# High and low parts of the last half key tiles share one product: nine products for a chunk instead of ten

## The chip, the core and the metric

The kernel runs on one core of a Trainium2 chip. Its time is the device time of one execution in microseconds (us), and the number that counts is the median of several runs. The engines are called PE (TensorE, matmuls), DVE (VectorE), ACT (ScalarE), POOL (GpSimd) and SP (SyncE, which issues DMAs here).

## The reference: what is computed

Attention with a threshold over 4 batches of 8 heads, 576 tokens and 64 columns a head, then two layers of a network over all 2304 tokens:

```python
scores = scale * q @ k.T                      # 576 x 576 for each head
thresh = max(scores) - tau                    # of each row
scores = where(scores >= thresh, scores, -1e9)
attn = softmax(scores)
x = attn @ v                                  # 576 x 64 for each head
x = relu(x @ w_in) ** 2 @ w_out               # 512 -> 2048 -> 512
h = x @ w2_in;  out = (h * tanh(softplus(h))) @ w2_out
```

## The kernel before

Numbers are float32. PE multiplies in a reduced form of it (`F32R`), so an operand is split: a high part, rounded to that form, and a low part, the rest. A product of two split operands is then three or four matmuls (high by high, high by low, and so on), all summed in PSUM.

**Slots.** The program is one list of slots, and every engine walks through it in order with its own share of each slot; semaphores tie them together. Two heads (a pair) have 9 query tiles of 128 rows, so there are 16 pairs and 144 tiles. Slot s computes the scores of tile s+1, the exponentials and the row maxima of tile s, the mask of tile s-1, and the transposes of tile s-3. From slot 40 on the first layer runs in the same slots: a slot has one `first_product` (12 matmuls, into the single PSUM tile `hidden`) and the `second_product` of the step two slots before (12 matmuls). The table `STEP_AT` leaves out one slot in nine, so in every nine slots there is one without a first product (slots 48, 57, 66, ..., 138; slot 39 has no product at all), called a **gap slot** here, and two slots later one without a second product (slots 50, 59, ..., 140, and slot 41 as the first of them), called a **half slot**.

**Order within a slot on PE:** transposes of tile s-3, first product, second product, scores, and in four slots of nine `weigh(c)`, the product of the transposed probabilities with the values for a chunk of 256 or 320 queries. There are 64 chunks, four to a pair. The first 16 (batch 0) go another way, with whole values in `weigh_whole`; the other 48 go through `weigh`. Both a gap slot and a half slot come right behind a slot that weighs a chunk of 256 queries.

**Transposed probabilities.** The 576 keys are covered by five tiles of 128 columns. The last but one holds keys 384 to 511 and the last keys 448 to 575, so that the lower 64 rows of the last tile repeat keys that the one before already has; the values for these rows are zero. PE transposes the five into one PSUM tile `pT`. ACT copies `pT` into the high part `pt_hi` (`high_probs`), then DVE subtracts it from `pT` into `pt_lo` (`low_probs`), 128x640 each. `transposes` of the next tile waits for that (`pT_low`), since it writes `pT` again. The values are split too, and `v_split` holds their high part in 64 columns and their low part in the next 64, so one matmul with `v_split` as the stationary operand gives both; the lower 64 rows of the result in `outs` belong to the high part and the upper 64 to the low part. ACT copies the upper ones to `o_low` (`move_low_rows`), DVE adds them (`sum_rows`) and SP stores the sum.

**Order on ACT in a slot:** the copy of `outs`, `high_probs`, `exponential`, in some slots the high parts of keys, queries and values, then `rectify` (`rg<-hidden` in the rows) and `high_square`, and sometimes `high_x`. `rectify` frees `hidden`: the next `first_product` waits for it (`relu_ready`). In a half slot ACT splits keys (`k_hi`) and values (`v_split`) ahead of `rectify`.

**Order on DVE:** row maxima (`s_neg`), `sum_rows`, mask (`probs<-s_neg,thresh,probs`), five small ones, `low_probs`, sometimes `low_x`.

In the rows, L562 is the helper of all ACT copies; L788 is `low_probs`, L796 `sum_rows`, L935 the transposes, L964 and L965 the two matmuls of `weigh`, L596 the exponential, L636 `rectify`, L642 `high_square`, L130 to L132 the three matmuls of each split product of the layers.

## Time and profile before

| | |
|---|---|
| median of 3 runs | 1150.06 us (1149.76 to 1151.54) |
| the profiled execution: its time, its span | 1150.88 us, 1149.1 us |
| mean granted TensorE clock | 0.994 of full speed |
| PE busy | 1105.6 us, 96% of the span |
| weight loads of PE | 1040.9 us, 91% |
| DVE, ACT, POOL busy | 759.2 us (66%), 645.4 us (56%), 586.2 us (51%) |
| PE's share of the chain that ended last | 86% |

A busy PE in this profile is not PE at its peak, since matmuls overlap in it: what a matmul costs is read from the distance between the starts of two that follow one another. The execution has three stages: batch 0 alone (to about 127 us), the other three batches beside the first layer (127 to 590 us), and the layers alone. The change bears on the second stage.

### The profile page before, as it was taken

The page shows a single profiled execution, that of the slowest core. Times are in us where ns is not written, and L with a number is a line of the kernel's source. Part 1 is how long each engine was busy: PE and PEld are TensorE (multiplying, and loading weights), DVE is VectorE, ACT ScalarE, POOL GpSimd, SP SyncE. Part 2 cuts the span into 40 slices and gives each one's busy share as a digit, 9 for nine tenths or more (in the row PEclk, how much of TensorE's full clock was granted, in tenths as well). Part 3 has the DMA queues.
Part 4 walks back from the last instruction along what each step waited for, and adds up shares of the span by engine and source line. Part 5 has one row for each costly group of instructions (what it writes and reads, how often), then busy time and mean ns, then how long its engine had stood idle before and what let it go on. Part 6 is the DMA issues. An engine that isn't in the chain of part 4 may idle for free.

```text
span 1149.1 us, 21018 instructions
## 1 busy us (share of the span) xinstructions
PE 1105.6 (96%) x7472; PEld 1040.9 (91%) x7472; DVE 759.2 (66%) x1977; ACT 645.4 (56%) x1230; POOL 586.2 (51%) x657
## 2 busy tenths in 40 slices
PE   5998899999999999999999999899999999999998
PEld 4776799999999999999999999889999999999997
DVE  5776677777677667676631014588787777878775
ACT  5786566665656566656543236555555555555554
POOL 5887788666766677676644445322222222222222
PEclk9999999999999999999999999999999999999999
DMA  5454322112222212121010204500101001010000
GB/s 147 130 153 113 92 74 72 53 49 70 55 71 58 60 47 81 44 69 53 20 50 11 92 2 146 156 19 1 56 1 56 1 1 56 1 55 1 28 1 28
DMA packets 73545, 65.33 MB, mean 57 GB/s; under 512 B 26080, under 2 KB 58848, under 8 KB 73440
## 3 DMA queue, kind: packets, MB, share of 16 engines
q1 hardware_dynamic: 68528, 58.98, 17.9%
q10 hardware_dynamic: 4912, 5.01, 1.3%
q8 instruction: 59, 0.97, 0.4%
q14 instruction: 46, 0.38, 0.1%
HBM read 49.81 MB, written 14.16 MB: 56 GB/s over the span
## 4 chain that ended last, share of the span: by engine, by line
PE 86%; DVE 4%; ACT 4%; issue 2%; DMA 2%; POOL 1%; SPq 0%; POOLq 0%; ACTq 0%; DVEq 0%
PE acc L130 8%; PE acc L131 8%; PE acc L132 8%; PE hidden L130 7%; PE hidden L132 7%; PE hidden L131 7%; PE pT L935 6%; PE scores L130 3%; PE scores L132 3%; PE scores L131 3%; PE pT L130 3%; PE pT L132 3%; PE pT L131 3%; PE outs L964 3%; PE outs L965 3%; PE scores L924 3%
## 5 line engine op out<-in xcount | busy, mean ns | idle before, releaser
L531 POOL TENSOR_TENSOR g_lo<-g,g_hi 128x384 fp32r<-128x384 f32 x96 | 97.9, 1020 | 314.0 <-ACT g_hi L562 314.0
L505 POOL TENSOR_SCALAR probs<-probs,inv_sum,flat 128x576 f32<-128x576 f32 x144 | 120.6, 839 | 130.8 <-DVE inv_sum L781 130.5
L130 PE MATMUL hidden<-x_hi,w_hi 128*128 128x256 f32 x576 | 170.6, 296 | 2.3 <-DVE x_lo L806 1.6
L130 PE MATMUL acc<-g_hi,w_hi 128*128 128x256 f32 x576 | 163.9, 285 | 0.2 <-POOL g_lo L526 0.2
L131 PE MATMUL acc<-g_lo,w_hi 128*128 128x256 f32 x576 | 162.9, 283 | 0.0
L132 PE MATMUL acc<-g_hi,w_lo 128*128 128x256 f32 x576 | 162.8, 283 | 0.0
L132 PE MATMUL hidden<-x_hi,w_lo 128*128 128x256 f32 x576 | 162.7, 282 | 0.0
L131 PE MATMUL hidden<-x_lo,w_hi 128*128 128x256 f32 x576 | 162.5, 282 | 0.0
L745 DVE TENSOR_SCALAR_CACHE_REDUCE s_neg<-scores 128x576 f32<-128x576 f32 x126 | 95.0, 754 | 71.5 <-PE scores L925 71.3
L521 POOL TENSOR_TENSOR rg<-rg 128x256 f32<-128x256 f32 x144 | 98.4, 683 | 75.4 <-ACT rg L636 74.5
L562 ACT ACTIVATE pt_hi<-pT 128x640 fp32r<-128x640 f32 x108 | 76.3, 707 | 71.0 <-PE pT L935 67.4
L596 ACT ACTIVATE probs<-s_neg,neg_top 128x576 f32<-128x576 f32 x144 | 110.5, 767 | 9.3 <-DVE s_neg L745 9.0
L562 ACT ACTIVATE g_hi<-g 128x384 fp32r<-128x384 f32 x96 | 50.5, 526 | 113.6 <-DVE g L847 113.6
L526 POOL TENSOR_TENSOR g_lo<-rg,g_hi 128x256 fp32r<-128x256 f32 x144 | 107.9, 749 | 11.3
L130 PEld LDWEIGHTS hidden<-x_hi,w_hi 128*128 128x128 f32 x576 | 109.8, 191 | 3.1 <-DVE x_lo L806 2.0
L935 PE MATMUL pT<-ident,probs 128*128 128x128 f32 x720 | 103.6, 275 | 9.3 <-DVE pt_lo L788 6.1
L130 PEld LDWEIGHTS acc<-g_hi,w_hi 128*128 128x128 f32 x576 | 110.4, 192 | 0.4 <-POOL g_lo L526 0.4
L131 PEld LDWEIGHTS acc<-g_lo,w_hi 128*128 128x128 f32 x576 | 110.5, 192 | 0.0
L132 PEld LDWEIGHTS acc<-g_hi,w_lo 128*128 128x128 f32 x576 | 110.4, 192 | 0.0
L131 PEld LDWEIGHTS hidden<-x_lo,w_hi 128*128 128x128 f32 x576 | 110.0, 191 | 0.0
L132 PEld LDWEIGHTS hidden<-x_hi,w_lo 128*128 128x128 f32 x576 | 109.7, 190 | 0.0
L935 PEld LDWEIGHTS pT<-ident,probs 128*128 128x128 f32 x720 | 84.3, 141 | 19.9 <-issue 9.8
(116 smaller groups left out, 3106.5 us busy)
## 6 DMA issues: line engine op xcount, KB each, us to landing
k_raw<-kT SPq DMA_DIRECT2D x64, 144.0 KB, 2.9
q_raw<-qT SPq DMA_DIRECT2D x62, 144.0 KB, 3.0
y<-w_in SPq DMA_DIRECT2D x26, 256.0 KB, 2.8
y<-w_out SPq DMA_DIRECT2D x26, 256.0 KB, 3.1
x_raw<-x SPq DMA_DIRECT2D x36, 128.0 KB, 2.1
x<-y ACTq DMA_DIRECT2D x9, 512.0 KB, 2.9
x_raw<-x SPq DMA_DIRECT2D x6, 768.0 KB, 5.1
out<-y SPq DMA_DIRECT2D x18, 256.0 KB, 2.4
```

The lines of the kernel that those rows point to most:

```text
L130: pe.matmul(out, a_hi, b_hi, start=first, stop=False, **flags)
L131: pe.matmul(out, a_hi, b_lo, start=False, stop=False, **flags)
L132: return pe.matmul(out, a_lo, b_hi, start=False, stop=last, **flags)
L505: pool.tensor_scalar(probs[:, t, :], probs[:, t, :], inv_sum[:, t:t + 1], flat[:, t:t + 1], ALU.mult, ALU.add).then_inc(probs_ready, 1)
L521: pool.tensor_tensor(g[:, i % 2, :], r[:, i % 2, :], r[:, i % 2, :], ALU.mult).then_inc(g_ready, 1)
L526: pool.tensor_tensor(g_lo[:, i % GRING1, :], g[:, i % 2, :], g_hi[:, i % GRING1, :].bitcast(F32), ALU.subtract).then_inc(g_split, 1)
L531: pool.tensor_tensor(g2_lo[:, k % GRING, :], g2[:, k % 2, :], g2_hi[:, k % GRING, :].bitcast(F32), ALU.subtract).then_inc(g2_split, 1)
L562: return act.activation(o, i, ACT.Copy)
L596: act.activation(probs[:, t, :], s_neg[:, n % 2, :], ACT.Exp, bias=neg_top[:, t:t + 1], scale=-1.0).then_inc(exp_ready, 1)
L745: dve.tensor_scalar(s_neg[:, n % 2, :].rearrange("p (c k) -> p c k", c=2), scores_of(n)[:, :, 0:HALF], -SCALE, None, ALU.mult, ALU.min, ac ...
L924: pe.matmul(out, q, k_hi[:, u, keys], start=(u, at) == parts[0], stop=False)
L935: mm = pe.transpose(pT[:, k * P:(k + 1) * P], probs[:, n % PRING, tile_at(k):tile_at(k) + P], ident[:, :])
```

## The change

From chunk 16 on the four matmuls of the last two key tiles become three. The fourth key tile is now the last one (keys 448 to 575, `BOTH`), the fifth keys 384 to 511 (`LAST`). The high part of `BOTH` is not multiplied any more, and neither is the low part of `LAST` as a tile; in their place one product takes a mixed tile, which has the low part of keys 384 to 447 in its lower 64 rows and the high part of keys 512 to 575 in its upper 64 rows, with a sixth block of values in the same order. For that:

- DVE writes `pt_lo` with two instructions, 128x512 and 64x128, instead of one of 128x640;
- ACT copies the upper 64 rows of the high part of `BOTH` into `pt_lo` (64x128), with a semaphore of its own, `pT_moved`, on which `weigh` waits; it first waits for its own copy to `pt_hi`;
- values have six blocks instead of five: ACT's and POOL's part of `v_split` are 128x384 instead of 128x320, and SP issues four DMAs a head for them instead of two;
- `o_low` and `o_sum` become `o_moved` and `o_sum` of 128 rows, in which the chunks take turns between lower and upper rows.

```diff
-                for k in range(QT):
-                    values = v_split[:, c // 2 % 2, k, :]
-                    pe.matmul(outs[:, 0:w], values, pt_hi[:, k, at:at + w], start=(k == 0), stop=False)
-                    mm = pe.matmul(outs[:, 0:w], values, pt_lo[:, k, at:at + w], start=False,
-                                   stop=(k == QT - 1))
+                for k, (_, place) in enumerate(KEY_TILES):
+                    values = v_split[:, c // 2 % 2, place, :]
+                    if k != BOTH:
+                        pe.matmul(outs[:, 0:w], values, pt_hi[:, k, at:at + w], start=(k == 0), stop=False)
+                    if k != LAST:
+                        pe.matmul(outs[:, 0:w], values, pt_lo[:, k, at:at + w], start=False, stop=False)
+
+                values = v_split[:, c // 2 % 2, QT, :]
+                mm = pe.matmul(outs[:, 0:w], values, pt_lo[:, LAST, at:at + w], start=False, stop=True)
                 mm.then_inc(out_ready, 1)
...
                 copy(pt_hi[:, :, at:at + P], pT_tile).then_inc(pT_high, 1)
+                if n == WHOLE_TILES:
+                    act.wait_ge(out_ready, WHOLE_CHUNKS)
+                act.wait_ge(pT_high, n + 1)
+                copy(pt_lo[HD:P, LAST, at:at + P], pt_hi[HD:P, BOTH, at:at + P].bitcast(F32)).then_inc(pT_moved, 1)
...
-                dve.tensor_tensor(pt_lo[:, :, at:at + P], pT_tile, pt_hi[:, :, at:at + P].bitcast(F32),
-                                  ALU.subtract).then_inc(pT_low, 1)
+                dve.tensor_tensor(pt_lo[:, 0:LAST, at:at + P], pT_tile[:, 0:LAST, :],
+                                  pt_hi[:, 0:LAST, at:at + P].bitcast(F32), ALU.subtract)
+                dve.tensor_tensor(pt_lo[0:HD, LAST, at:at + P], pT_tile[0:HD, LAST, :],
+                                  pt_hi[0:HD, LAST, at:at + P].bitcast(F32), ALU.subtract).then_inc(pT_low, 1)
...
-                copy(v_split[:, h % 2, :, 0:HD], v_raw[:, h % 2, 0:QT, :]).then_inc(v_high, 1)
+                copy(v_split[:, h % 2, :, 0:HD], v_raw[:, h % 2, :, :]).then_inc(v_high, 1)
...
-                sp.dma_start(v_raw[HD:P, h % 2, QT - 1, :], v[h * SEQ + 512:(h + 1) * SEQ, :]
-                             ).then_inc(v_loaded[h % 2], 16)
+                if h < HEADS:
+                    sp.dma_start(v_raw[HD:P, h % 2, QT - 1, :], v[h * SEQ + 512:(h + 1) * SEQ, :]
+                                 ).then_inc(v_loaded[h % 2], 16)
+                else:
+                    sp.dma_start(v_raw[:, h % 2, QT - 1, :], v[h * SEQ + 448:(h + 1) * SEQ, :]
+                                 ).then_inc(v_loaded[h % 2], 16)
+                    sp.dma_start(v_raw[0:HD, h % 2, QT, :], v[h * SEQ + 384:h * SEQ + 448, :]
+                                 ).then_inc(v_loaded[h % 2], 16)
+                    sp.dma_start(v_raw[HD:P, h % 2, QT, :], v[h * SEQ + 512:(h + 1) * SEQ, :]
+                                 ).then_inc(v_loaded[h % 2], 16)
```

What ACT has to do in a half slot (slot 59), before; the line numbers of the changed program are other ones, L562 becomes L586, L596 becomes L620, L636 and L642 become L664 and L670:

```order
L562 ACTIVATE o_low<-outs 64x256
L562 ACTIVATE pt_hi<-pT 128x5x128
L596 ACTIVATE probs<-s_neg,neg_top 128x576
L562 ACTIVATE k_hi<-k_raw 128x576
L562 ACTIVATE v_split<-v_raw 128x5x64
L636 ACTIVATE rg<-hidden 128x256
L642 ACTIVATE g_hi<-rg 128x256
```

And the same slot on ACT in the changed kernel:

```order
L586 ACTIVATE o_moved<-outs 64x256
L586 ACTIVATE pt_hi<-pT 128x5x128
L586 ACTIVATE pt_lo<-pt_hi 64x128
L620 ACTIVATE probs<-s_neg,neg_top 128x576
L586 ACTIVATE k_hi<-k_raw 128x576
L586 ACTIVATE v_split<-v_raw 128x6x64
L664 ACTIVATE rg<-hidden 128x256
L670 ACTIVATE g_hi<-rg 128x256
```

One instruction more stands between `pt_hi` and the exponential, ahead of `rg<-hidden`, and `v_split` is longer.

PE in a slot that weighs a chunk of 256, from `weigh` to the transposes behind it, before:

```order
L964 MATMUL outs<-pt_hi,v_split 128x256
L965 MATMUL outs<-pt_lo,v_split 128x256
L964 MATMUL outs<-pt_hi,v_split 128x256
L965 MATMUL outs<-pt_lo,v_split 128x256
L964 MATMUL outs<-pt_hi,v_split 128x256
L965 MATMUL outs<-pt_lo,v_split 128x256
L964 MATMUL outs<-pt_hi,v_split 128x256
L965 MATMUL outs<-pt_lo,v_split 128x256
L964 MATMUL outs<-pt_hi,v_split 128x256
L965 MATMUL outs<-pt_lo,v_split 128x256
L935 MATMUL pT<-ident,probs 128x128 x5
```

And in the changed kernel, where L1001 is the product of the mixed tile:

```order
L996 MATMUL outs<-pt_hi,v_split 128x256
L998 MATMUL outs<-pt_lo,v_split 128x256
L996 MATMUL outs<-pt_hi,v_split 128x256
L998 MATMUL outs<-pt_lo,v_split 128x256
L996 MATMUL outs<-pt_hi,v_split 128x256
L998 MATMUL outs<-pt_lo,v_split 128x256 x2
L996 MATMUL outs<-pt_hi,v_split 128x256
L1001 MATMUL outs<-pt_lo,v_split 128x256
L965 MATMUL pT<-ident,probs 128x128 x5
```

Nine instead of ten, and nothing else on PE changes its place.

## Rows read from the trace of the kernel before

**Rows 1.** Engines in the second stage: length, then busy us and instructions of each
```profile
127.00:590.00 463.00, 456.40 (x3736) 451.62 (x3735) 322.86 (x1012) 280.55 (x548) 325.90 (x370) 1.00 0.21 57
```

**Rows 2.** What PE waited for in that stage: us in total, times, longest
```profile
PE pT L935 <- DVE pt_lo L788: 5.4, 13, 0.4
```

**Rows 3.** Timeline of PE, from the weighing in slot 58 through half slot 59
```profile
207.28 0.28 PE L964 MATMUL outs<-pt_hi,v_split 128*128 128x256 f32 x1
...
208.47 0.71 PE L935 MATMUL pT<-ident,probs 128*128 128x128 f32 x5
...
211.56 0.74 PE L935 MATMUL pT<-ident,probs 128*128 128x128 f32 x5 [0.43 <-DVE pt_lo L788]
212.05 0.36 PE L130 MATMUL hidden<-x_hi,w_hi 128*128 128x256 f32 x1
```

**Rows 4.** Timeline of PE: a chunk of 320 and the transposes behind it
```profile
307.00 0.31 PE L964 MATMUL outs<-pt_hi,v_split 128*128 128x320 f32 x1
...
308.46 0.71 PE L935 MATMUL pT<-ident,probs 128*128 128x128 f32 x5
```

**Rows 5.** Timeline of ACT in half slot 59
```profile
209.21 0.70 ACT L562 ACTIVATE pt_hi<-pT 128x640 fp32r<-128x640 f32 x1 [0.17 <-PE pT L935]
209.82 0.76 ACT L596 ACTIVATE probs<-s_neg,neg_top 128x576 f32<-128x576 f32 x1
...
211.06 0.46 ACT L562 ACTIVATE v_split<-v_raw 128x320 fp32r<-128x320 f32 x1
211.42 0.37 ACT L636 ACTIVATE rg<-hidden 128x256 f32<-128x256 f32 x1
211.82 0.42 ACT L642 ACTIVATE g_hi<-rg 128x256 fp32r<-128x256 f32 x1
```

**Rows 6.** Timeline of DVE in half slot 59
```profile
210.60 0.81 DVE L788 TENSOR_TENSOR pt_lo<-pT,pt_hi 128x640 fp32r<-128x640 f32 x1
211.33 0.75 DVE L745 TENSOR_SCALAR_CACHE_REDUCE s_neg<-scores 128x576 f32<-128x576 f32 x1
```

**Rows 7.** Groups by line and shape, second stage: busy us, mean ns
```profile
L499 POOL TENSOR_TENSOR v_split<-v_raw,v_split 128x320 fp32r<-128x320 f32 x23 | 29.8, 1296 | 0.9
...
L796 DVE TENSOR_TENSOR o_sum<-outs,o_low 64x320 f32<-64x320 f32 x24 | 11.6, 483 | 29.6 <-ACT o_low L562 29.6
L562 ACT ACTIVATE v_split<-v_raw 128x320 fp32r<-128x320 f32 x23 | 10.6, 459 | 0.0
...
L562 ACT ACTIVATE x_hi<-x_raw 128x256 fp32r<-128x256 f32 x24 | 9.7, 402 | 0.0
L796 DVE TENSOR_TENSOR o_sum<-outs,o_low 64x256 f32<-64x256 f32 x23 | 9.6, 417 | 20.9 <-ACT o_low L562 20.9
```

**Rows 8.** Timeline of gap slot 57: transposes, the low part, the next transposes
```profile
200.23 0.71 PE L935 MATMUL pT<-ident,probs 128*128 128x128 f32 x5
...
202.37 0.81 DVE L788 TENSOR_TENSOR pt_lo<-pT,pt_hi 128x640 fp32r<-128x640 f32 x1
...
203.32 0.74 PE L935 MATMUL pT<-ident,probs 128*128 128x128 f32 x5
```

**Rows 9.** Timelines of ACT and PE, end of half slot 41
```profile
132.77 0.37 ACT L636 ACTIVATE rg<-hidden 128x256 f32<-128x256 f32 x1
...
133.28 0.36 PE L130 MATMUL hidden<-x_hi,w_hi 128*128 128x256 f32 x1 [0.58 <-ACT rg L636]
```

**Rows 10.** Timelines of DVE and PE around the end of slot 53
```profile
184.30 0.81 DVE L788 TENSOR_TENSOR pt_lo<-pT,pt_hi 128x640 fp32r<-128x640 f32 x1
...
185.78 0.71 PE L935 MATMUL pT<-ident,probs 128*128 128x128 f32 x5
```

**Rows 11.** Timelines of ACT and PE around the end of slot 55
```profile
194.12 0.37 ACT L636 ACTIVATE rg<-hidden 128x256 f32<-128x256 f32 x1
...
195.57 0.36 PE L130 MATMUL hidden<-x_hi,w_hi 128*128 128x256 f32 x1
```

**Rows 12.** Instructions on v_raw: duration ns min/median/max, first and last start
```profile
L364 SPq DMA_DIRECT2D v_raw<-v x32: 511/517/813, 3.1 to 527.8; - x32
```

More of the change, by code:

```diff
@@ L66 @@
 SLOTS = BEGIN2 + NB * FT + LEAD + 1
-def tile_at(k):
-    return min(k * P, SEQ - P)
+KEY_TILES = [(0, 0), (P, 1), (2 * P, 2), (SEQ - P, 4), (3 * P, 3)]
+BOTH, LAST = 3, 4
 def chunk_ended(n):
@@ L175, in attention_and_layers @@
         k_lo = early("k_lo", [P, 2, SEQ], F32R)
-        v_split = early("v_split", [P, 2, QT, 2 * HD], F32R)
+        v_split = early("v_split", [P, 2, QT + 1, 2 * HD], F32R)
         s_neg = early("s_neg", [P, 2, SEQ])
         probs = early("probs", [P, PRING, SEQ])
-        o_low = early("o_low", [HD, 320])
-        o_sum = early("o_sum", [HD, 2, 320])
+        o_moved = early("o_moved", [P, 320])
+        o_sum = early("o_sum", [P, 320])
         ident = early("ident", [P, P])
@@ L235, in scores_of, with rows_of, other_rows @@
             return both_acc if n < WHOLE_TILES and n % 2 else scores
+        def rows_of(c):
+            return slice(c % 2 * HD, (c % 2 + 1) * HD)
+        def other_rows(c):
+            return slice((c + 1) % 2 * HD, ((c + 1) % 2 + 1) * HD)
         def outs_of(c):
@@ L279, in attention_and_layers @@
         pT_low = sem("pT_low")
+        pT_moved = sem("pT_moved")
         out_ready = sem("out_ready")
-        low_moved = sem("low_moved")
+        rows_moved = sem("rows_moved")
         out_summed = sem("out_summed")
@@ L318, in w_tile, with values_loaded @@
             return w[:, f * 2 * DM:(f + 1) * 2 * DM]
+        def values_loaded(h):
+            return 32 * (h // 2 + 1) + 32 * max(0, (h - HEADS) // 2 + 1)
         def query_columns(h):
@@ L371, in store @@
                 at = h // HEADS * SEQ
-                o = o_sum[:, c % 2, :]
+                o = o_sum[rows_of(c), :]
                 if c % 4 == 0:
@@ L498, in split_values @@
                 pool.wait_ge(v_high, h + 1 - HEADS)
-                pool.tensor_tensor(v_split[:, h % 2, :, HD:2 * HD], v_raw[:, h % 2, 0:QT, :],
+                pool.tensor_tensor(v_split[:, h % 2, :, HD:2 * HD], v_raw[:, h % 2, :, :],
                                    v_split[:, h % 2, :, 0:HD].bitcast(F32), ALU.subtract).then_inc(v_ready, 1)
@@ L622, in move_low_rows @@
                 act.wait_ge(out_summed, c)
-                copy(o_low[:, 0:w], outs[HD:P, 0:w]).then_inc(low_moved, 1)
+                copy(o_moved[rows_of(c), 0:w], outs[other_rows(c), 0:w]).then_inc(rows_moved, 1)
             def copy_rows(c):
@@ L629, in copy_rows @@
                 act.wait_ge(out_ready, c + 1)
-                copy(o_sum[:, c % 2, 0:w], outs_of(c)[0:HD, 0:w]).then_inc(out_summed, 1)
+                copy(o_sum[rows_of(c), 0:w], outs_of(c)[0:HD, 0:w]).then_inc(out_summed, 1)
             def rectify(i):
@@ L700, in _ @@
                 if c is not None and c >= WHOLE_CHUNKS:
[L701 removed]
+                    move_rows(c)
                 if 0 <= s - LAG < WHOLE_TILES:
@@ L794, in sum_rows @@
                     dve.wait_ge(stored[c % 2], stored_up_to(c - 1, c % 2))
-                dve.wait_ge(low_moved, c + 1 - WHOLE_CHUNKS)
-                dve.tensor_tensor(o_sum[:, c % 2, 0:w], outs[0:HD, 0:w], o_low[:, 0:w], ALU.add
+                dve.wait_ge(rows_moved, c + 1 - WHOLE_CHUNKS)
+                dve.tensor_tensor(o_sum[rows_of(c), 0:w], outs[rows_of(c), 0:w], o_moved[rows_of(c), 0:w], ALU.add
                                   ).then_inc(out_summed, 1)
@@ L933, in transposes @@
                     pe.wait_ge(pT_low, n - WHOLE_TILES)
-                for k in range(QT):
-                    mm = pe.transpose(pT[:, k * P:(k + 1) * P],
-                                      probs[:, n % PRING, tile_at(k):tile_at(k) + P], ident[:, :])
+                for k, (key, _) in enumerate(KEY_TILES):
+                    mm = pe.transpose(pT[:, k * P:(k + 1) * P], probs[:, n % PRING, key:key + P], ident[:, :])
                 mm.then_inc(pT_ready, 1)
@@ L951, in weigh_whole @@
                 for k in keys:
-                    mm = pe.matmul(outs_of(c)[:, 0:w], values[:, k * HD:k * HD + P], pt_whole[c % 2][:, k, 0:w],
+                    at = KEY_TILES[k][1] * HD
+                    mm = pe.matmul(outs_of(c)[:, 0:w], values[:, at:at + P], pt_whole[c % 2][:, k, 0:w],
                                    start=(k == 0), stop=(k == QT - 1))
@@ L960, in weigh @@
                 pe.wait_ge(pT_low, PER * (c // 4) + last + 1 - WHOLE_TILES)
+                pe.wait_ge(pT_moved, PER * (c // 4) + last + 1 - WHOLE_TILES)
                 pe.wait_ge(v_ready, c // 2 + 1 - HEADS)
-                for k in range(QT):
-                    values = v_split[:, c // 2 % 2, k, :]
-                    pe.matmul(outs[:, 0:w], values, pt_hi[:, k, at:at + w], start=(k == 0), stop=False)
-                    mm = pe.matmul(outs[:, 0:w], values, pt_lo[:, k, at:at + w], start=False,
-                                   stop=(k == QT - 1))
+                for k, (_, place) in enumerate(KEY_TILES):
[6 more added lines that the diff above has]
+                mm = pe.matmul(outs[:, 0:w], values, pt_lo[:, LAST, at:at + w], start=False, stop=True)
                 mm.then_inc(out_ready, 1)
```

7 lines of the change are left out of this document (3 added, 4 removed).

## The prediction, made before the changed kernel ran

> **What bounds the kernel now.** I read the busy time by stage first. In the second stage PE is busy for 456.4 of 463.0 us [rows 1], with the granted clock at 1.00, while DVE (322.9), ACT (280.6) and POOL (325.9) have a third of it free. So PE's own work sets the pace. The waits come next: PE waits 5.4 us in 13 places for the low part `pt_lo` of the transposed probabilities [rows 2], 0.43 us in each of the 12 half slots as in [rows 3], 5.2 us together, and 0.2 once more. Last the timelines, which show what stands beside PE in the places where it doesn't set the pace. There are two kinds. In a half slot PE has no second product, and its transposes start only when `pt_lo` has ended: 210.60 + 0.81 = 211.41 [rows 6], transposes at 211.56 [rows 3], 0.15 us later, of which I take 0.14 as the way of a semaphore. In a gap slot it is the same without a recorded wait: `pt_lo` ends at 202.37 + 0.81 = 203.18, transposes at 203.32, again 0.14 us later [rows 8]. In both, the chain runs from the end of the weighing before (ACT copies `outs`, DVE adds, masks, and then subtracts), so its start moves with the weighing, and a shorter weighing is kept. A longer `pt_lo` is paid in full there. In all other slots PE is alone on the path.
>
> **What is saved.** One of ten products of `weigh`, 48 times. With 256 columns ten take 208.47 - 207.28 = 1.19 us [rows 3], 0.119 us each; with 320 columns 308.46 - 307.00 = 1.46 us [rows 4], 0.146 each. 24 chunks of each: 24 x 0.119 + 24 x 0.146 = 2.86 + 3.50 = 6.36 us. The nine have the same shapes, and each has its own weight load as before.
>
> **What DVE pays.** 640 columns in one instruction become 512 and 128 in two. The fixed part of a DVE subtraction or addition with a PSUM operand follows from `o_sum`: 417 ns at 256 columns, 483 at 320 [rows 7], so 1.03 ns a column and 153 ns fixed. The 64x128 one then takes 0.285 us and the 128x512 one 0.81 - 0.13 = 0.68. Two that follow each other overlap: `pt_lo` starts at 210.60, takes 0.81, and the next starts at 211.33 [rows 6], 0.08 us before its end. The pair takes 0.68 - 0.08 + 0.285 = 0.88 us instead of 0.81; with the exact halves (133 ns less for 128 columns) it is 0.06 to 0.07. I take 0.06. Bounds: 0 (a perfect overlap of the fixed part) and 0.153 (none). In the gap slots it is paid in full, 12 times with slot 39: 0.72 us. In the other slots it is hidden. The closest I found away from the two kinds is the end of slot 53, where `pt_lo` ends at 185.11 and the transposes start at 185.78 [rows 10], 0.53 us more than the semaphore needs.
>
 By that rule the gap slots would lose 12 x 0.125 = 1.5 us instead of 0.7, and the overlap in the trace speaks for the smaller value.
>
> **What ACT pays.** Every tile gets a copy of 64x128 from SBUF to SBUF. Its length from the two nearest rows: 402 ns at 256 columns (`x_hi`), 459 at 320 (`v_split`) [rows 7], so 0.89 ns a column and 402 - 114 = 288 ns; I take 0.29. It also waits for the copy to `pt_hi` ahead of it, and that ends the overlap: `pt_hi` starts at 209.21 and takes 0.70, the exponential starts at 209.82, 0.09 to 0.10 us before its end [rows 5]. With the wait the next starts 0.03 us after the end, as `g_hi` behind `rg` shows (211.42 + 0.37 = 211.79, start 211.82) [rows 5]. So the exponential and all behind it in the slot come 0.10 + 0.03 + 0.29 - 0.10 = 0.32 to 0.33 us later. In a half slot `v_split` is longer by 64 columns too, 0.055 us. Together 0.385 us.
>
> Who waits for that? In the half slot ACT works without a gap from `pt_hi` at 209.21 to the end of `rg` at 211.79 [rows 5], and the next first product needs `rg` to free `hidden`. It starts at 212.05 [rows 3]. That is 0.26 us after `rg`; from slot 41, where PE did wait for `rg`, such a start needs 0.14 (132.77 + 0.37 = 133.14, start 133.28) [rows 9]. So only 0.12 us of the 0.385 are free, and the first product starts 0.265 us later than now. This takes the place of the 0.06 of DVE there: the transposes come 0.06 later, but the first product behind them waits for `rg` anyway. In slot 41, which is late already, all of 0.385 is paid. 11 x 0.265 + 0.39 = 3.3 us. (The last, slot 140, has no keys to split, but a copy and low part of x before the next row maxima; I price it like the others.)
>
> In other slots the copy is hidden. The tightest after these is the end of slot 55: `rg` ends at 194.49, the first product starts at 195.57 [rows 11], 0.94 us more than 0.14. The exponential itself is needed by the mask one slot later.
>
> **What else moves.** POOL's part of `v_split` goes from 1.30 us [rows 7] to an estimated 1.56 for a fifth more columns; what it holds up is a square whose low part is due two slots later, and POOL is idle for a third of the stage. SP issues two DMAs more for each of 24 heads at 0.52 us [rows 12], so about 1 us later for what is behind them, in a queue that works one to three slots (3 us and more each) ahead. `o_moved` in place of `o_low` has the same shapes. The new wait of `weigh` on `pT_moved` is for an instruction near the start of the slot at whose end `weigh` stands, and earlier than the `pt_lo` for which it waits already. I cost these at nothing. Without their cover, a late POOL or SP would show as a wait of PE for `g_lo` or of ACT for a DMA.
>
> **The sum.** -6.36 + 0.72 + 3.3 = -2.3 us. The profiled execution took 1150.88 us, span 1149.1; it would take 1148.5, span 1146.8. The median shown is 0.8 us below the profiled time, so the median to come is 1150.06 - 2.3 = **1147.7 us**.
>
> **Rivals.**
> 1. *The saving is nearly whole.* If ACT's new copy were free in the half slots (shorter or overlapping, so that the delay stays under 0.12 us), only DVE's part is lost, 24 x 0.06 = 1.4 us: -4.9 us, 1145.1. For it: ACT is busy for 61% of the stage only. Against it: it has no gap in just these slots. With the copy at the least its rows allow, 402 - 256 x 0.89 = 174 ns (no time for its columns), the delay is 0.21 + 0.055, the loss there 0.145 x 11 + 0.27 = 1.9, and the sum -3.8: 1146.3.
> 2. *DVE's second instruction costs its whole fixed part,* 0.125 to 0.153 us. In the half slots the wait for `rg` covers it, in the gap slots it costs 12 x 0.09 = 1.1 us more at most: -1.2 us, 1148.8. The rule quoted above gives this case, at 12 x 0.065 = 0.8 us more, 1148.5.
> 3. *Slower: ACT's copy is as long as that of the whole tile.* If reading what was just written makes the 64x128 copy as long as `pt_hi`, 0.70 us, the delay in a half slot is 0.10 + 0.03 + 0.70 - 0.10 + 0.055 = 0.785, PE waits 0.665 longer in 11 and 0.785 in one: 8.1 + 0.7 - 6.36 = +2.4 us, 1152.5. It breaks even where 11 x (d - 0.12) + d = 5.64, at a delay d of 0.58 us, so at a copy of 0.49 us. For it: nothing in the trace is exactly this copy. Against it: all ACT copies follow one line by columns.
> 4. *PE saves nothing,* because nine products with the same output are not faster than ten. Nothing speaks for it, since their starts are evenly spaced and next in line is always a matmul.
>
> **How the numbers follow.** About 0.2% (2.3 us) is what a measurement of this kernel can tell from no change. My forecast lies just on that edge. Forecast (-1.6 to -3.1) 0.62; rival 1 0.14 (whole or in part); rival 2 0.12; rival 3 and everything else that makes ACT or a queue late 0.10; rival 4 0.02. The forecast's own range is 1147.0 to 1148.5. The range for 8 in 10 goes to rival 1 below and past rival 2 above: 1145.2 to 1149.6. Faster by over 0.2% is half of the forecast, rival 1 and nothing else, with a little more because parts of what I charge may overlap: 0.48. Within 0.2%: 0.45. Slower by over 0.2%: 0.07, from rival 3.
>
> **What would show it.** In the changed profile: `weigh` takes 9 x 0.119 and 9 x 0.146 us from its first start to the next transposes; `pt_lo` lasts 0.68 and 0.285 us, the second start some 0.6 after the first; ACT's new copy lasts 0.29 and the exponential starts about 0.93 us after `pt_hi` instead of 0.61. PE has a wait for `rg` in each of the 12 half slots, 0.2 us beyond its transposes and more in slot 41, where today there is one in all. From the transposes of a half slot to the next first product it is 3.84 us instead of 3.58 (212.05 - 208.47); from transposes to transposes in a gap slot 3.15 instead of 3.09. What makes me wrong: a new copy of another length, a chain that DVE finds late for another reason, above all its mask, which shares a slot with POOL's work, or a wait in a slot where I see none.

## The result, and the profile after

| | before | changed kernel |
|---|---|---|
| median | 1149.92 us (1149.23 to 1151.54, 6 runs) | 1156.02 us (1154.86 to 1157.84, 6 runs) |
| the profiled execution: its time, its span | 1150.88, 1149.1 | 1157.50, 1155.7 |

The ratio is 1.0048, with an interval of 1.0034 to 1.0062: the change makes the kernel 0.5% slower, where 0.2% faster was forecast. The one rival with that sign, a copy on ACT as long as that of the whole tile, isn't the reason either: the copy is as short as predicted.

The busy time by stage, as in [rows 1]; the middle line is the second stage.

```profile
0.00:127.00 127.00, 101.68 (x534) 81.74 (x534) 82.10 (x323) 86.58 (x138) 92.56 (x94) 0.97 0.48 135
127.00:590.00 463.00, 448.92 (x3637) 439.99 (x3637) 339.62 (x1122) 317.09 (x647) 325.27 (x366) 1.00 0.22 60
590.00:1155.70 565.70, 554.87 (x3256) 513.76 (x3254) 354.36 (x641) 282.91 (x555) 168.69 (x197) 1.00 0.12 39
```

In 463 us PE was busy for 456.4 us before and is for 448.9 now, with the clock at 1.00 in both. So PE waits more, and DVE (339.6 instead of 322.9) and ACT (317.1 instead of 280.6) work more. What PE waits for, as in [rows 2]: us in total, times, longest.

```profile
PE pT L965 <- POOL probs L529: 8.4, 23, 0.5
PE outs L996 <- issue: 3.0, 6, 0.5
PE hidden L134 <- ACT rg L664: 1.1, 1, 1.1
PE hidden L134 <- DVE x_lo L836: 0.8, 1, 0.8
PE pT L965 <- DVE pt_lo L818: 0.8, 1, 0.8
```

The 13 waits of the transposes have become 24. The first line names POOL, but its probabilities belong to the next tile's transposes as much as `pt_lo` does, both end close together, and the transposes start 0.15 us behind the end of `pt_lo`, as before. The wait for `rg` that the prediction announced for every half slot shows in one slot alone: in the others the transposes ahead of it are recorded as busy until the first product starts, so the delay shows only in the distance between starts. The second line is new in kind: `weigh` itself waits, in six places.

The lengths that the prediction used, by groups from 127 to 596 us, the end of the stage's last slots (busy us, mean ns | idle before):

```profile
L798 DVE SCALAR_TENSOR_TENSOR probs<-s_neg,thresh,probs 128x576 f32<-128x576 f32 x105 | 108.6, 1034 | 0.7
...
L816 DVE TENSOR_TENSOR pt_lo<-pT,pt_hi 128x512 fp32r<-128x512 f32 x107 | 72.5, 677 | 4.2 <-ACT pt_hi L586 3.5
L586 ACT ACTIVATE pt_lo<-pt_hi 64x128 fp32r<-64x128 f32 x107 | 32.9, 308 | 3.4
L523 POOL TENSOR_TENSOR v_split<-v_raw,v_split 128x384 fp32r<-128x384 f32 x23 | 29.9, 1300 | 0.9
L818 DVE TENSOR_TENSOR pt_lo<-pT,pt_hi 64x128 fp32r<-64x128 f32 x107 | 29.1, 272 | 0.0
```

ACT's copy takes 0.308 us (0.29 predicted), DVE's pair 0.677 and 0.272 (0.68 and 0.285). The surprise is the mask, which the change doesn't touch: 1.034 us on average, where it was 0.924.

**Where the time went, by slot.** I measured every slot from its transposes to the next, in both traces. From slot 39 to slot 146, the last with transposes, the sum is 6.2 us longer; slot 39 itself came 1.6 us later in this execution, and the rest of the span differs by 1.2 the other way. In us, by kinds of slots (slots after 48, with two typical lengths):

| slots | before, after | sum of the difference |
|---|---|---|
| half slot | 3.09, 3.14 | +0.5 |
| the slot behind it | 3.97, 4.25 | +3.1 |
| the next one, weighs 320 (11 slots) | 5.40, 5.25; but 6.03 in slots 52, 70, 88, 106, 124 | +2.2 |
| the other three kinds that weigh | 5.15, 5.04; 5.40, 5.25; 5.12, 5.00 | -3.9 |
| gap slot (10) | 3.09, 3.41 | +3.0 |
| the two kinds left | 3.94, 3.94 | +0.1 |
| slots 39 to 48 | | +1.2 |

The products are saved as predicted (0.12 and 0.15 us a chunk), and the half slots cost about what was predicted. Two rows are not as predicted: the gap slots, 0.32 us longer and not 0.06, and five slots in which 0.15 is not gained and 0.63 is lost.

**A gap slot.** Slot 66 in the kernel before, timeline of DVE and PE:

```profile
239.32 0.71 PE L935 MATMUL pT<-ident,probs 128*128 128x128 f32 x5
240.00 0.42 DVE L796 TENSOR_TENSOR o_sum<-outs,o_low 64x256 f32<-64x256 f32 x1 [0.90 <-ACT o_low L562]
240.34 0.80 DVE L770 SCALAR_TENSOR_TENSOR probs<-s_neg,thresh,probs 128x576 f32<-128x576 f32 x1
241.37 0.17 DVE L781 RECIPROCAL inv_sum<-safe_sum 128x1 f32<-128x1 f32 x1
241.45 0.81 DVE L788 TENSOR_TENSOR pt_lo<-pT,pt_hi 128x640 fp32r<-128x640 f32 x1
```

The same slot in the changed kernel:

```profile
242.81 0.71 PE L965 MATMUL pT<-ident,probs 128*128 128x128 f32 x5
243.49 0.43 DVE L826 TENSOR_TENSOR o_sum<-outs,o_moved 64x256 f32<-64x256 f32 x1 [0.78 <-ACT o_moved L586]
243.95 0.82 DVE L798 SCALAR_TENSOR_TENSOR probs<-s_neg,thresh,probs 128x576 f32<-128x576 f32 x1
245.00 0.17 DVE L809 RECIPROCAL inv_sum<-safe_sum 128x1 f32<-128x1 f32 x1
245.20 0.69 DVE L816 TENSOR_TENSOR pt_lo<-pT,pt_hi 128x512 fp32r<-128x512 f32 x1
245.81 0.27 DVE L818 TENSOR_TENSOR pt_lo<-pT,pt_hi 64x128 fp32r<-64x128 f32 x1
246.22 0.74 PE L965 MATMUL pT<-ident,probs 128*128 128x128 f32 x5 [0.22 <-POOL probs L529]
```

The mask starts 0.46 us behind the start of the addition instead of 0.34, and `pt_lo` 0.20 behind the reciprocal instead of 0.08. Both are 0.12 us, with no wait of DVE in the rows, and only where the addition works in the upper rows (odd chunks, as in every gap slot); behind even chunks the mask follows at 0.34 as before. With 0.06 for the pair and some hundredths in the masks and starts that is the 0.32. Put against the ends of the instructions ahead: before, the mask starts 0.08 us before the addition has ended (240.42) and `pt_lo` 0.09 before the reciprocal has (241.54); now both start 0.03 us behind such an end (243.92, 245.17).

**One of the five.** Slot 70 before, DVE and POOL:

```profile
254.12 0.74 POOL L526 TENSOR_TENSOR g_lo<-rg,g_hi 128x256 fp32r<-128x256 f32 x1
254.43 0.70 DVE L806 TENSOR_TENSOR x_lo<-x_raw,x_hi 128x256 fp32r<-128x256 f32 x1 [0.59 <-ACT x_hi L562]
254.63 0.71 PE L935 MATMUL pT<-ident,probs 128*128 128x128 f32 x5
...
255.73 0.81 DVE L770 SCALAR_TENSOR_TENSOR probs<-s_neg,thresh,probs 128x576 f32<-128x576 f32 x1
...
255.92 1.92 POOL L494 TENSOR_TENSOR q_split<-q_raw,q_split 64x576 fp32r<-64x576 f32 x1
...
258.56 0.31 PE L964 MATMUL outs<-pt_hi,v_split 128*128 128x320 f32 x1
```

And after:

```profile
258.64 0.71 PE L965 MATMUL pT<-ident,probs 128*128 128x128 f32 x5
...
258.92 0.42 DVE L836 TENSOR_TENSOR x_lo<-x_raw,x_hi 128x256 fp32r<-128x256 f32 x1 [1.21 <-ACT x_hi L586]
...
259.94 2.07 DVE L798 SCALAR_TENSOR_TENSOR probs<-s_neg,thresh,probs 128x576 f32<-128x576 f32 x1
259.96 1.43 POOL L518 TENSOR_TENSOR q_split<-q_raw,q_split 64x576 fp32r<-64x576 f32 x1
...
262.91 0.27 DVE L818 TENSOR_TENSOR pt_lo<-pT,pt_hi 64x128 fp32r<-64x128 f32 x1
...
263.28 0.39 PE L996 MATMUL outs<-pt_hi,v_split 128*128 128x320 f32 x1 [0.55 <-issue]
```

The mask starts 1.30 us behind the transposes instead of 1.10, because ACT, later by its copy, delivers `x_hi` later, and so DVE `x_lo` and the row maxima. `x_lo` starts 0.48 us later (0.28 behind the transposes, where it was 0.20 ahead of them), but only 0.20 of it reaches the mask: before, `x_lo` took 0.70 us beside POOL's `g_lo`, now it takes 0.42. Before, the mask was 0.19 us ahead of POOL's `q_split` and took 0.81 us, while POOL took 1.92. Now they start together, POOL takes 1.43 and the mask 2.07. It ends 0.62 us behind POOL's end (259.96 + 1.43 = 261.39; 259.94 + 2.07 = 262.01), as if it had 0.62 us of work to do from there. `pt_lo` then ends at 263.18, and `weigh` of this slot, which needs it, starts at 263.28.

### The profile page after: what moved, and what is told of

The parts are those of the page before. It is cut to its first block, busy times and chain, and to the rows that moved or that the text cites. A ratio compares the mean times of both kernels' runs of the same rounds, so it can differ in the third digit from the quotient of the medians.

```text
span 1155.7 us, 21235 instructions
## 1 busy us (share of the span) xinstructions
PE 1105.5 (96%) x7424; PEld 1035.5 (90%) x7424; DVE 776.1 (67%) x2085; ACT 686.6 (59%) x1338; POOL 586.5 (51%) x657
## 4 chain that ended last, share of the span: by engine, by line
PE 81%; DVE 5%; ACT 5%; POOL 4%; issue 3%; DMA 2%; SPq 0%; POOLq 0%; ACTq 0%; DVEq 0%
PE acc L134 7%; PE acc L135 7%; PE acc L136 7%; PE hidden L134 7%; PE hidden L136 7%; PE hidden L135 7%; PE pT L965 5%; PE pT L136 3%; PE pT L134 3%; PE pT L135 3%; PE scores L136 3%; PE scores L134 3%; PE scores L135 3%; PE outs L996 2%; PE outs L998 2%
## 5 line engine op out<-in xcount | busy, mean ns | idle before, releaser
L586 ACT ACTIVATE g_hi<-g 128x384 fp32r<-128x384 f32 x96 | 50.5, 526 | 113.6 <-DVE g L877 113.6
L620 ACT ACTIVATE probs<-s_neg,neg_top 128x576 f32<-128x576 f32 x144 | 111.6, 775 | 10.1 <-DVE s_neg L773 7.1
L798 DVE SCALAR_TENSOR_TENSOR probs<-s_neg,thresh,probs 128x576 f32<-128x576 f32 x108 | 111.2, 1030 | 0.7
L586 ACT ACTIVATE pt_hi<-pT 128x640 fp32r<-128x640 f32 x108 | 76.0, 703 | 52.9 <-PE pT L965 49.7
```

Source lines behind the costliest of these rows:

```text
L586: return act.activation(o, i, ACT.Copy)
L620: act.activation(probs[:, t, :], s_neg[:, n % 2, :], ACT.Exp, bias=neg_top[:, t:t + 1], scale=-1.0).then_inc(exp_ready, 1)
L798: dve.scalar_tensor_tensor(out=probs[:, t, :], in0=s_neg[:, n % 2, :], scalar=thresh[:, t:t + 1], in1=probs[:, t, :], op0=ALU.is_le, op1=A ...
```

## The experiments

All ratios are to the kernel before, run beside it on the same chip, and can differ a little from the quotient of the two medians. Sums over the second stage are made like those above (6.2 us in the changed kernel), from one profiled execution each; whole times scatter by 1 to 5 us between executions. Where an expectation speaks of a type, it means the number of the slot modulo nine: the gap slots are of type 3, the half slots of type 5, the slot behind them of type 6, the five long slots of type 7.

**1. Nine products alone**, on the kernel before. The low part of the last key tile is left out of the values' product, so the kernel does less than the reference asks.

```diff
-                    pe.matmul(outs[:, 0:w], values, pt_hi[:, k, at:at + w], start=(k == 0), stop=False)
-                    mm = pe.matmul(outs[:, 0:w], values, pt_lo[:, k, at:at + w], start=False,
+                    mm = pe.matmul(outs[:, 0:w], values, pt_hi[:, k, at:at + w], start=(k == 0),
                                    stop=(k == QT - 1))
+                    if k < QT - 1:
+                        pe.matmul(outs[:, 0:w], values, pt_lo[:, k, at:at + w], start=False, stop=False)
```

> The kernel before, with nine products a chunk from chunk 16 on and nothing else changed: the product with the low part of the last key tile is left out (so the output lacks that part). If a product costs what the starts of its neighbours show (0.119 us at 256 columns, 0.146 at 320), 48 of them save 6.4 us, 1143.5 us. If nine are not faster than ten, or a stall takes the place, 1149.9.

Measured: 1144.19 us against 1151.49, ratio 0.9938 [0.9925, 0.9952], stage sum -6.15. Slot 48 is 0.22 us longer in it (its mask takes 1.15 us instead of 0.92, beside POOL's work) and the others are 6.37 shorter, so the saving of 6.36 is right, and all of the loss is on the other side.

**2. The sum always in the lower rows**, in the changed kernel; all sums then share one buffer, so each addition waits for the store of the chunk before.

```diff
-            return slice(c % 2 * HD, (c % 2 + 1) * HD)
+            odd = c % 2 if c < WHOLE_CHUNKS else 0
+            return slice(odd * HD, (odd + 1) * HD)
...
-                if c >= 2:
-                    dve.wait_ge(stored[c % 2], stored_up_to(c - 1, c % 2))
+                for parity in range(2):
+                    dve.wait_ge(stored[parity], stored_up_to(c, parity))
```

> The changed kernel, but from chunk 16 on o_moved and o_sum always in the lower 64 rows (one buffer each, the sum waits for the store of the chunk before). Theory A, that a DVE addition on the upper 64 rows makes the instructions behind it later (mask 0.12 us, low part 0.11 us), which is paid in the 12 gap slots: 2.8 us less than the changed kernel, 1153.2 us, and gap slots 3.15 us long instead of 3.41. Theory B, that the gap slots are longer by the second DVE instruction or POOL: no change, 1156.0.

Measured: 1155.56 us, ratio 1.0034 [1.0021, 1.0046], stage sum +4.2 instead of +6.2. Gap slots take 3.17 instead of 3.41; nothing else moves much. So the rows of the addition cost 2 us, and the rest of the loss isn't theirs.

**3. ACT's copy late**, behind `rg`, `g_hi` and `x_hi` of its slot.

```diff
                 copy(pt_hi[:, :, at:at + P], pT_tile).then_inc(pT_high, 1)
+
+            def move_high(n):
+                at = COLUMN[n % PER]
...
                 if s in SPLIT_AT:
                     high_x(*SPLIT_AT[s])
+                if WHOLE_TILES <= s - LAG < TILES:
+                    move_high(s - LAG)
```

> The changed kernel with ACT's new 64x128 copy moved to the end of its share of the slot, behind rg, g_hi and x_hi. Theory A, that its place ahead of the exponential costs 0.33 us in each half slot (3.6 with slot 41) and, by making x_hi late, 0.78 us in each of five slots of type 7 of nine (3.9): 7.6 us less than the changed kernel, 1148.4 us. Theory B, that the place of the copy costs only the half slots and the five slots are long for another reason (POOL's longer value split, DMAs): 1152.4.

Measured: 1156.53 us, ratio 1.0044 [1.0031, 1.0056], stage sum +5.85. The half slots keep their 3.14 us, and the slots behind them are at 3.97 again as before the change, 3 us back. But the other kind of slot that weighs 320 queries (slots 54, 63, ..., 144) loses 0.28 us (5.53 instead of 5.25, eleven times): `weigh` needs the copy, which now ends 3.88 us behind the transposes in slot 63, and starts at 4.13 instead of 3.94, and slots 52 and 70 still take 6.15. My expectation took the copy's cover in the weighing slots for granted, and it isn't there: a step moved out of one slot kind landed on the path in another.

**4. `high_x` ahead of the queries' high part** on ACT, in the slots before the five, in the changed kernel.

```diff
+                if s in SPLIT_AT and s % PER == 6:
+                    high_x(*SPLIT_AT[s])
                 if s in QUERIES_AT:
                     high_queries(QUERIES_AT[s])
...
-                if s in SPLIT_AT:
+                if s in SPLIT_AT and s % PER != 6:
                     high_x(*SPLIT_AT[s])
```

> The changed kernel with high_x taken ahead of q_split on ACT in the slots of type 6 of nine alone. Theory A, that in five slots of type 7 the mask starts just as POOL's q_split does and lasts 2.07 us instead of 0.81 because x_hi, x_lo and the row maxima came 0.4 us later: the five long slots (6.03 us) go back to 5.25, 3.9 us less than the changed kernel, 1152.1. Theory B, that the long mask has to do with POOL or the DMAs of the values: no change, 1156.0.

Measured: 1152.53 us, ratio 1.0009 [1.0000, 1.0018], stage sum +2.4. The five slots take 5.25, all others what they took in the changed kernel. The masks start 0.17 to 0.23 us ahead of `q_split` again and take 0.81 us.

**5. The alternate rows alone**, on the kernel before (`o_low` and `o_sum` of 128 rows, odd chunks in the upper 64).

```diff
-                copy(o_low[:, 0:w], outs[HD:P, 0:w]).then_inc(low_moved, 1)
+                copy(o_low[rows_of(c), 0:w], outs[other_rows(c), 0:w]).then_inc(low_moved, 1)
...
-                dve.tensor_tensor(o_sum[:, c % 2, 0:w], outs[0:HD, 0:w], o_low[:, 0:w], ALU.add
+                dve.tensor_tensor(o_sum[rows_of(c), 0:w], outs[rows_of(c), 0:w], o_low[rows_of(c), 0:w], ALU.add
```

> The kernel before with one part of the change alone: o_low and o_sum hold 128 rows and the chunks take turns between lower and upper rows. Theory A (an addition on the upper rows delays what follows on DVE by 0.12 and 0.11 us, which 12 gap slots pay in full): +2.8 us against before, gap slots 3.32 us instead of 3.09. Theory B (only together with the second DVE instruction): no change.

Measured: 1155.85 us against 1151.44, ratio 1.0037 [1.0025, 1.0049], stage sum +3.8, of it 2.5 in ten gap slots (3.35), 0.8 in slot 48 and 0.5 in slots 40 and 45.

**6. ACT's copy alone**, on the kernel before, into a block of values that nothing reads.

```diff
                 copy(pt_hi[:, :, at:at + P], pT_tile).then_inc(pT_high, 1)
+                if n == WHOLE_TILES:
+                    act.wait_ge(out_ready, WHOLE_CHUNKS)
+                act.wait_ge(pT_high, n + 1)
+                copy(v_raw[HD:P, :, QT, :], pt_hi[HD:P, QT - 1, at:at + P].bitcast(F32).rearrange("p (a d) -> p a d", a=2))
```

> The kernel before with ACT's 64x128 copy of every tile alone, written to a block of v_raw that nobody reads any more. By the prediction's own sum the half slots pay 0.33 - 0.12 = 0.21 us each, 2.6 us in all. Theory A adds to that the late x_hi, which lets five masks coincide with POOL's q_split, up to 0.8 us each: 2.6 to 6.6 us. Theory B (the five slots have another cause): 2.6 us and no long slot of type 7.

Measured: 1156.35 us, ratio 1.0049 [1.0037, 1.0061], stage sum +5.4: +2.8 behind the half slots (4.25), +2.1 in the same five slots, 5.84 instead of 5.40, and +0.5 in slots 39 to 48. The copy alone brings both of its losses, 5 us and not 3.3. The second one comes about in another way than in the changed kernel. Slot 70, whose transposes start at 257.43, POOL and DVE:

```profile
257.48 0.82 POOL L505 TENSOR_SCALAR probs<-probs,inv_sum,flat 128x576 f32<-128x576 f32 x1
257.68 0.90 DVE L810 TENSOR_TENSOR x_lo<-x_raw,x_hi 128x256 fp32r<-128x256 f32 x1 [1.20 <-ACT x_hi L562]
...
259.18 1.31 DVE L774 SCALAR_TENSOR_TENSOR probs<-s_neg,thresh,probs 128x576 f32<-128x576 f32 x1
```

Here it is `x_lo` that comes together with POOL's work, and it takes 0.90 us instead of 0.42. The mask then starts 1.75 us behind the transposes, when POOL has been at `q_split` for 0.79 us, and takes 1.31.

**7. The low part in two instructions alone** (128x512 and 128x128), on the kernel before.

```diff
-                dve.tensor_tensor(pt_lo[:, :, at:at + P], pT_tile, pt_hi[:, :, at:at + P].bitcast(F32),
-                                  ALU.subtract).then_inc(pT_low, 1)
+                dve.tensor_tensor(pt_lo[:, 0:QT - 1, at:at + P], pT_tile[:, 0:QT - 1, :],
+                                  pt_hi[:, 0:QT - 1, at:at + P].bitcast(F32), ALU.subtract)
+                dve.tensor_tensor(pt_lo[:, QT - 1, at:at + P], pT_tile[:, QT - 1, :],
+                                  pt_hi[:, QT - 1, at:at + P].bitcast(F32), ALU.subtract).then_inc(pT_low, 1)
```

> The kernel before with low_probs in two instructions, 128x512 and 128x128, and nothing else. Both theories: 0.055 us in each of the 12 gap and 12 half slots, where transposes wait for it, +1.3 us. If the second instruction costs a whole fixed part (0.125 us or more), +3 us.

Measured: 1153.33 us, ratio 1.0017 [1.0008, 1.0025], stage sum +1.4: 0.06 us in each gap slot (3.15) and each half slot (3.15), as priced, but for slots 57 and 120, which take 3.28.

**8. and 9. Which rows?** Two halves of experiment 5 on the kernel before: only the output of odd sums in the upper rows, and only their inputs.

```diff
-                dve.tensor_tensor(o_sum[:, c % 2, 0:w], outs[0:HD, 0:w], o_low[:, 0:w], ALU.add
+                dve.tensor_tensor(o_sum[rows_of(c), 0:w], outs[0:HD, 0:w], o_low[0:HD, 0:w], ALU.add
...
-                dve.tensor_tensor(o_sum[:, c % 2, 0:w], outs[0:HD, 0:w], o_low[:, 0:w], ALU.add
+                dve.tensor_tensor(o_sum[sum_at(c), 0:w], outs[rows_of(c), 0:w], o_low[rows_of(c), 0:w], ALU.add
```

(`sum_at` gives the lower rows from the second batch on; in that half the addition also waits for the store of the chunk before.)

> The kernel before with the sum of odd chunks written to the upper 64 rows, and both inputs of the addition in the lower ones. If the delay behind the addition comes from where it writes, 12 gap slots are 3.35 us long as with all operands in the upper rows (3 to 4 us more than before); if it comes from where it reads, 3.09 us and no change.

> The kernel before with both inputs of the addition in the upper 64 rows for odd chunks, and the output always in the lower ones (one buffer, so the sum waits for the store of the chunk before). If the delay comes from where it reads, gap slots are 3.35 us long and the kernel is 3 to 4 us slower than before; if from where it writes, 3.09 to 3.12.

Measured: the output alone 1153.94 us against 1151.73, ratio 1.0015 [1.0007, 1.0024], stage sum +2.2, gap slots 3.22; the inputs alone 1154.50, ratio 1.0028 [1.0017, 1.0039], stage sum +4.4, gap slots 3.38. The expectations took it for one or the other; it is both. Slot 66 with only the output in the upper rows:

```profile
242.39 0.42 DVE L802 TENSOR_TENSOR o_sum<-outs,o_low 64x256 f32<-64x256 f32 x1 [0.90 <-ACT o_low L568]
242.84 0.82 DVE L776 SCALAR_TENSOR_TENSOR probs<-s_neg,thresh,probs 128x576 f32<-128x576 f32 x1
243.89 0.16 DVE L787 RECIPROCAL inv_sum<-safe_sum 128x1 f32<-128x1 f32 x1
243.97 0.80 DVE L794 TENSOR_TENSOR pt_lo<-pT,pt_hi 128x640 fp32r<-128x640 f32 x1
```

And with only the inputs there:

```profile
241.55 0.43 DVE L805 TENSOR_TENSOR o_sum<-outs,o_low 64x256 f32<-64x256 f32 x1 [0.92 <-ACT o_low L571]
242.01 0.82 DVE L779 SCALAR_TENSOR_TENSOR probs<-s_neg,thresh,probs 128x576 f32<-128x576 f32 x1
243.05 0.17 DVE L790 RECIPROCAL inv_sum<-safe_sum 128x1 f32<-128x1 f32 x1
243.25 0.82 DVE L797 TENSOR_TENSOR pt_lo<-pT,pt_hi 128x640 fp32r<-128x640 f32 x1
```

Both delay the mask (0.45 instead of 0.34 behind the addition). Only the inputs delay `pt_lo` too (0.20 instead of 0.08 behind the reciprocal). Between the two stand the mask and five small instructions, all in SBUF alone, and `pt_lo` is the next to read PSUM after the addition read its upper rows.

**10. POOL's low part of the queries later**, the changed kernel with one move on POOL: in the slots before the five, behind the square and its low part.

```diff
-                if s in QUERIES_AT:
+                if s in QUERIES_AT and s % PER != 6:
                     split_queries(QUERIES_AT[s], s)
...
                     low_square(i)
+                if s in QUERIES_AT and s % PER == 6:
+                    if i is not None:
+                        pool.wait_ge(g_split, i + 1)
+                    split_queries(QUERIES_AT[s], s)
```

> The changed kernel with one move on POOL alone: in the slots ahead of the five long ones POOL's low part of the queries (q_split, 1.43 us beside the mask of 2.07 us) stands behind the square and its low part instead of ahead of them. Nothing of ACT or DVE changes, so x_hi, x_lo and the row maxima come as late as in the changed kernel. If POOL's q_split holds the mask: the mask beside it goes from 2.07 to 0.8 us, or to 1.2 to 1.4 if the square of 0.6 us holds it instead (the mask would then end some 0.6 us behind the end of the square), and in both cases the low parts end in time, the five slots go from 6.03 to 5.25 us, the stage's sum from +6.2 to about +2.3 and the time to about 1152.5. If the mask is long for what DVE or ACT do (a late x_lo, the exponential): it stays at 2.07, the five slots at 6.03, and the time at 1156.

Measured: 1153.92 us against 1152.04, ratio 1.0016 [1.0007, 1.0026], stage sum +2.8 (+2.3 expected; 0.3 of the rest lies in slot 39). Slot 70, POOL and DVE:

```profile
258.28 0.71 PE L969 MATMUL pT<-ident,probs 128*128 128x128 f32 x5
...
259.49 0.61 POOL L545 TENSOR_TENSOR rg<-rg 128x256 f32<-128x256 f32 x1
...
259.57 1.14 DVE L802 SCALAR_TENSOR_TENSOR probs<-s_neg,thresh,probs 128x576 f32<-128x576 f32 x1
...
260.18 1.14 POOL L550 TENSOR_TENSOR g_lo<-rg,g_hi 128x256 fp32r<-128x256 f32 x1
...
263.53 0.71 PE L969 MATMUL pT<-ident,probs 128*128 128x128 f32 x5
```

The mask is as late as in the changed kernel (1.29 us behind the transposes), but takes 1.14, and again ends 0.61 us behind a POOL instruction, now the square (259.49 + 0.61 = 260.10; 259.57 + 1.14 = 260.71). POOL's next, `g_lo`, takes 1.14 instead of some 0.74 and ends 0.61 behind the mask. All five slots take 5.25.

**11. and 12. The better version.** From what the runs showed: the sum in the lower rows (experiment 2), and ACT's copy behind `pt_hi` only in slots that weigh, else behind `high_x`; the second kernel has experiment 4's order too.

```diff
                     high_probs(s - LAG)
+                    if weighing_at(s) is not None:
+                        move_high(s - LAG)
...
                     high_x(*SPLIT_AT[s])
+                if WHOLE_TILES <= s - LAG < TILES and weighing_at(s) is None:
+                    move_high(s - LAG)
```

> The changed kernel with the lower rows of the earlier run, and with ACT's copy placed by slot: right behind pt_hi in slots that weigh a chunk (where weigh waits for it), behind rg, g_hi and x_hi in all others. Theory A: half slots 3.97 us again instead of 4.25 (3.5 us), gap slots 3.17 (2.4 us), slots of type 0 at 5.25, and the five slots of type 7 back to 5.25 (3.9 us) if x_hi is early enough for the mask: 9.8 us less than the changed kernel, 1146.2; if some masks still coincide with q_split, up to 1150. Theory B (a nine-product kernel can't be faster with the copy on ACT at all): 1150 or more.

> The placed copy and lower rows together with high_x ahead of q_split in slots of type 6. The trace of the placed copy alone has no long mask beside q_split any more, so if that was all that x_hi did, this is the same, within 0.1%. If the long masks are a matter of luck from execution to execution, it is faster by some of 0.8 us for each that is avoided.

Measured: 1147.53 us against 1151.44, ratio 0.9974 [0.9964, 0.9984], and 1147.42 against 1151.73, ratio 0.9954 [0.9942, 0.9967]. The stage sums are alike, -3.2 in both, so the second move adds nothing once the copy is out of the way. Half slots are 3.17 and the slots behind them 3.97, gap slots 3.17, all weighing slots 5.25 or less. This is faster than both kernels.

## Why the prediction was wrong

**The saving.** Right: 6.36 predicted, 6.15 measured alone, and 6.37 without slot 48 (experiment 1).

**DVE's pair.** Right: 0.06 us in a gap slot predicted, 0.06 measured (experiment 7). The estimate of 0.125 us that the prediction worked out from the Trainium skill is too high here.

**ACT's copy in the half slots.** Right in mechanism and nearly in size, by two errors against each other. From the transposes to the next first product it is 3.90 us (212.05 to 215.95), 0.32 longer and not 0.265. The exponential comes 1.07 us behind `pt_hi` instead of the 0.93 predicted: it starts 0.02 behind the end of the copy, where I had given it the overlap of 0.10 again, and the copy starts 0.04 behind `pt_hi`. The way from the end of `rg` to the product is 0.06 us, and not the 0.14 of slot 41 [rows 9]:

```profile
212.05 0.71 PE L965 MATMUL pT<-ident,probs 128*128 128x128 f32 x5
...
212.79 0.70 ACT L586 ACTIVATE pt_hi<-pT 128x640 fp32r<-128x640 f32 x1 [0.17 <-PE pT L965]
...
213.53 0.31 ACT L586 ACTIVATE pt_lo<-pt_hi 64x128 fp32r<-64x128 f32 x1
...
213.86 0.78 ACT L620 ACTIVATE probs<-s_neg,neg_top 128x576 f32<-128x576 f32 x1
...
215.53 0.36 ACT L664 ACTIVATE rg<-hidden 128x256 f32<-128x256 f32 x1
...
215.95 0.38 PE L134 MATMUL hidden<-x_hi,w_hi 128*128 128x256 f32 x1
```

These are ACT and PE in half slot 59. For the half slots and those behind them it makes +3.6 us, where 2.9 had been counted, so this term of the sum was 0.7 too small.

**Failed step: "`o_moved` in place of `o_low` has the same shapes ... I cost these at nothing."** The shapes are the same, the rows are not. An addition in the upper rows delays the mask behind it by 0.11 to 0.12 us, and, by its inputs, `pt_lo` by as much again: 0.25 us in each of ten gap slots, 3.8 us in all where it is alone (experiment 5, with slots 40, 45 and 48), 2 us in the changed kernel (experiment 2). The Trainium skill has a rule for it in VectorE: DVE Perf Modes, Two Vector instructions with no wait between them: an instruction whose output or inputs start in another group of 32 partitions than the last write or read of the same memory starts only when every earlier Vector instruction has finished. The traces agree: the mask and `pt_lo` start 0.03 us behind the end of the instruction ahead, where they started 0.08 or 0.09 before it, and experiments 8 and 9 show it for output and inputs apart. The price, 0.11 to 0.12 us, is from these runs. The prediction weighed another rule of that page and left this one out.

**Failed step: "In other slots the copy is hidden."** I looked at whether PE waits for `rg`, and found 0.94 us of room. The path that had no room went another way: ACT's `x_hi`, DVE's `x_lo`, the row maxima, the mask. The mask came only 0.2 us later, but that moved the mask from just ahead of POOL's `q_split` to together with it, and such a pair doesn't share: 1.26 us for the mask, 0.78 for PE (6.03 instead of 5.25), 5 times, 3.9 us. The prediction named "above all its mask, which shares a slot with POOL's work" as what would make it wrong, and gave it no price, though the rows were there: in the kernel before, `q_split` takes 1.87 to 1.92 us beside the mask and 1.43 elsewhere. Experiments 4 and 10 show the cause from both sides: with the mask 0.2 us earlier, or with POOL's instruction moved away and the mask as late as ever, the five slots take 5.25.

**Slots 39 to 48.** +1.2 us, where the prediction comes to about 0 (0.5 of losses, and as much saved by four chunks). Slot 40 is 0.7 longer, since the first product waits 0.8 for `x_lo` (the waits above); in the better version, with the copy placed late there, it is 0.15. Slot 48 is 0.75 longer: two of the delays by rows, and the mask beside POOL's low part of the weights, 1.38 us instead of 0.92.

**The sum.** The stage came out 8.5 us longer than predicted (+6.2 instead of -2.3): 3.9 in the five slots, 2.4 in the gap slots, 1.2 in slots 39 to 48, 0.7 in and behind the half slots, and 0.3 in small ones. Experiments 1, 5, 6 and 7 add up to -6.15 + 3.8 + 5.4 + 1.4 = +4.4 us, against +6.2 for all together. The remaining 1.8 is mainly the five slots, where the copy alone costs 0.44 each and the whole change 0.78: in experiment 6 it is `x_lo` that is held first (0.90 us) and the mask starts in the middle of `q_split`, in the changed kernel `x_lo` is free (0.42) and the mask starts just with `q_split`. What `x_lo` meets is POOL's scaling of the probabilities, which starts 0.20 us ahead of it in the one and 0.12 in the other, where the scaling is the one stretched (1.08 us instead of 0.82). POOL works there without a gap from `k_lo` on, and its part of `v_split` takes 1.54 us in the changed kernel instead of 1.40, so the values' longer split, which the prediction put at nothing, is the likely reason; it was not tried alone.

Open is why the mask starts 0.12 us late in a few gap slots behind an addition in the lower rows: slots 57 and 120 in experiments 2, 7, 11 and 12, and slot 93 in the kernel before and in experiments 1 and 6.

## What to carry to other kernels

A new short instruction costs more than its length: where an engine hands over several things in a slot, follow each of them to its last reader, and ask for every one how far it may slip before it meets another engine's work. If two instructions on DVE and POOL already stretch each other in the trace, their start times belong in the prediction, since 0.2 us decided here whether POOL's `q_split` was held for 0.5 us, which cost nothing, or the mask for 1.26. And a buffer in other rows isn't the same buffer: compare start rows, not only shapes, of neighbouring DVE instructions.

## What the runs showed of the hardware

**A DVE instruction with two inputs in SBUF and a POOL instruction on SBUF exclude each other.** In the second stage of the changed kernel the mask is over 0.95 us long 26 times, and each time it ends 0.61 to 0.62 us behind the end of a POOL subtraction; in the kernel before 20 times, with the same distance. Where `x_lo` is held, it ends 0.27 to 0.28 us behind POOL's instruction (0.70 us beside `g_lo`, 0.90 beside the scaling of the probabilities, 0.42 alone). The 36 masks of batch 0, which read the scores from PSUM and have one other input in SBUF, take 0.80 to 0.82 us in both kernels, though 20 of them before and 17 now stand beside a POOL subtraction. POOL is held in turn where the mask is first: `q_split` 1.92 instead of 1.43 us. The Trainium skill says this in SBUF — State Buffer, SBUF: two separate sides: the two engines share a pair of ports, whoever is first has it for the whole instruction, and the other is blocked. What I hadn't expected is how finely it turns, and that a recorded start isn't yet the holding of the ports. Over the second stages of all kernels run, the mask was held beside `q_split` when it started up to 0.03 us ahead of it, and `q_split` was held from 0.07 us on (experiment 6: 2.04 us beside a mask of 0.81). Beside other POOL instructions both outcomes occur between 0 and 0.06 us.

**Rows of DVE instructions.** The 0.12 us of a change of rows is no wait in the profile and no longer instruction: it shows only in the distance between two starts. The later instruction starts 0.03 us behind the end of the one ahead, and not 0.08 us before it.
